# Attention, squared-ReLU layer and gated layer on one core: both layers by one level of Strassen, weights streamed from DRAM

## The reference

```python
k_p = k.reshape(B, H, Sp, 8, D).mean(axis=3); v_p = the same of v     # B, H, S, D = 8, 8, 576, 64; Sp = 72
attn = softmax(scale * q @ k_p.T) @ v_p                               # softmax over the 72 pooled keys
x = attn.transpose(0, 2, 1, 3).reshape(4608, 512)                     # 8 batches of 576 tokens
h = x @ moe_w_in                                                      # 512 x 2048
x2 = (s * relu(h) ** 2 + b) @ moe_w_out                               # 2048 x 512
h2 = x2 @ moe2_w_in                                                   # 512 x 2048
out = (h2 * sigmoid(h2)) @ moe2_w_out                                 # 2048 x 512
```

## Time and profile before

| what | value |
|---|---|
| median of 3 runs | 1729.53 us (1729.25 to 1729.66) |
| span of the profiled execution, first to last instruction | 1729.0 us |
| TensorE matmul busy | 1702.6 us, 98% |
| VectorE busy | 752.9 us, 44% |
| ScalarE busy | 568.8 us, 33% |
| GpSimd busy | 280.7 us, 16% |
| moved by DMA | 75.88 MB, 44 GB/s over the span |

### The profile page before, as it was taken

How to read it: one execution, slowest core, us unless ns; L and a number is a source line. 1 busy time by engine, 2 the same in 40 slices (tenths; PEclk the granted TensorE clock), 3 DMA queues, 4 the chain that set the end, 5 groups by cost and what they waited for, 6 DMA issues and landing times.

```text
span 1729.0 us, 22661 instructions
## 1 busy us (share of the span) xinstructions
PE 1702.6 (98%) x7894; PEld 1416.9 (82%) x7894; DVE 752.9 (44%) x1248; ACT 568.8 (33%) x1099; POOL 280.7 (16%) x374
## 2 busy tenths in 40 slices
PE   7999999999999999999999999999999999999999
PEld 6777888888888888888888888888888888888887
DVE  6666555555655555552345232323232323232322
ACT  4444333333334334332323232323232323232222
POOL 5652211222121121200077000000000000000000
PEclk9999999999999999999999999999999999999999
DMA  5431111111111111120123010101010101010000
GB/s 154 129 104 54 44 54 35 42 59 36 60 42 29 59 42 45 36 74 1 49 91 127 1 49 0 49 0 49 0 49 0 49 0 49 0 49 0 24 0 24
DMA packets 30509, 75.88 MB, mean 44 GB/s; under 512 B 7824, under 2 KB 7824, under 8 KB 27024
## 3 DMA queue, kind: packets, MB, share of 16 engines
q1 hardware_dynamic: 22848, 55.59, 10.5%
q10 hardware_dynamic: 7632, 19.93, 3.0%
HBM read 55.58 MB, written 19.92 MB: 44 GB/s over the span
## 4 chain that ended last, share of the span: by engine, by line
PE 90%; DVE 5%; issue 2%; ACT 2%; DMA 1%; POOL 0%; SPq 0%; ACTq 0%; DVEq 0%; POOLq 0%
PE y_ps L525 43%; PE h_ps L512 42%; PE a_ps L473 2%; PE a_ps L487 2%; PE a_ps L456 1%; DVE g_raw L799 1%; DVE rowmax L739 1%; ACT act L629 1%; ACT g_hi L639 1%; DVE rowsum L754 1%; DVE g_lo L811 0%; DVE probs L761 0%; DVE probs L749 0%; DMA xrest_dram<-xrest 0%; DMA x_raw<-kT 0%
## 5 line engine op out<-in xcount | busy, mean ns | idle before, releaser
L512 PE MATMUL h_ps<-x_hi,w_hi 128*128 128x512 f32 x1152 | 453.8, 394 | 4.3 <-DVE x_lo L787 3.7
L525 PE MATMUL y_ps<-g_hi,w_hi 128*128 128x512 f32 x1152 | 452.6, 393 | 0.0
L512 PE MATMUL h_ps<-x_hi,w_lo 128*128 128x512 f32 x1152 | 450.2, 391 | 0.0
L512 PE MATMUL h_ps<-x_lo,w_hi 128*128 128x512 f32 x1152 | 449.9, 391 | 0.0
L525 PE MATMUL y_ps<-g_hi,w_lo 128*128 128x512 f32 x1152 | 449.4, 390 | 0.0
L525 PE MATMUL y_ps<-g_lo,w_hi 128*128 128x512 f32 x1152 | 448.8, 390 | 0.0
L629 ACT ACTIVATE act<-h_ps 128x512 f32<-128x512 f32 x288 | 171.9, 597 | 679.2 <-PE h_ps L512 679.1
L796 DVE TENSOR_TENSOR g_raw<-h_ps,act 128x512 f32<-128x512 f32 x144 | 99.5, 691 | 411.3 <-ACT act L629 411.2
L512 PEld LDWEIGHTS h_ps<-x_hi,w_hi 128*128 128x128 f32 x1152 | 217.1, 188 | 48.2 <-issue 4.1
L512 PEld LDWEIGHTS h_ps<-x_hi,w_lo 128*128 128x128 f32 x1152 | 216.7, 188 | 45.8
L525 PEld LDWEIGHTS y_ps<-g_hi,w_lo 128*128 128x128 f32 x1152 | 216.3, 188 | 45.8
(11 more groups left out here) (106 smaller groups left out, 977.5 us busy)
## 6 DMA issues: line engine op xcount, KB each, us to landing
w_stage<-weights SPq DMA_DIRECT2D x64, 256.0 KB, 2.9
x_dram<-y_out ACTq DMA_DIRECT2D x9, 1024.0 KB, 3.9
x_raw<-x_dram SPq DMA_DIRECT2D x9, 1024.0 KB, 4.7
k_stage<-kT SPq DMA_DIRECT2D x30, 288.0 KB, 3.2
q_sb<-qT SPq DMA_DIRECT2D x30, 288.0 KB, 2.8
v_stage<-vP SPq DMA_DIRECT2D x30, 288.0 KB
out<-y_out ACTq DMA_DIRECT2D x8, 1024.0 KB, 3.9
xrest_dram<-xrest ACTq DMA_DIRECT2D x32, 32.0 KB, 1.6
```

What stands on the lines that cost most here:

```text
L512: last = nc.tensor.matmul(h_ps[f % 2][:, :], w[:, f, cols], x[:, c, :], start=(c == 0 and n == 0), stop=(c == KC - 1 and n == 2))
L525: last = nc.tensor.matmul(y_ps[m][:, :], w[:, f, cols], g[:, f % G, :], start=(f == 0 and n == 0), stop=(f == FS - 1 and n == 2))
```

## The change

One level of Strassen's scheme (in a form with operand sums T1 to T4) replaces each layer product of 2x2 quadrants, 8 block products, by 7. A unit is now one batch of 576 columns in two halves of 288 (`TH`). It goes through the first layer (an even phase `ph`) and then the second (odd), before the next batch; there are 8 units and 16 phases. A phase has 56 slots: 28 up (4 groups `g` of 7 products) and 28 down (7 products in 2 pieces of 2 slots; `d` is the slot counted from the first down slot). Each slot is 12 matmuls of 288 columns and uses one granule of weights, 128 x 1024 float32 with high and low parts. Granules are no longer kept in SBUF: a ring of 6 is loaded from `w_dram`, one per slot, in every phase. `w_dram` is filled by the kernel: 32 sets of raw weights (`load_set`, 512 KB) are summed by GpSimd (`sum_set`, 4 operations on 128x256), split by ScalarE and VectorE (`prep`, in two parts of 4x256 and 3x256 columns), and stored by SyncE (`store_set`, two DMAs that write 1 KB pieces, 1.84 MB in all). Sets 0 to 3 are made ahead of the first slot, the other 28 during slots 0 to 76 of the first unit.

In the core of each step, PSUM sums are copied by ScalarE (`part_up`, `part_down`) and combined by VectorE (`form`); the results of the function are kept in float32 for the whole phase (`gq`), where VectorE makes the operand sums (`combine`, `xsum`), ScalarE the high parts (`dhi`, `xhi`) and VectorE the low parts (`dlo`, `xlo`). The attention of batch u+1 is woven into unit u: for units 1 to 6 wholly into the 56 slots of the even phase, 14 slots for each pair.

The diff in its core; the rest is names, buffers and the matching changes of SyncE's and GpSimd's lists:

```diff
-NB = 512
+ORDER = ("P1", "P5", "P6", "P3", "P7", "P2", "P4")
+TH = 288
+DOWN = ((0, 0), (1, 0), (0, 1), (1, 1), (2, 0), (2, 1), (3, 0), (3, 1), (4, 0), (4, 1), (5, 0), (5, 1), (6, 0), (6, 1))
+PIECES = tuple(2 if i < 4 else 1 for i in range(len(DOWN)))
+RING = 6
...
+TURN_NAMES = ("scores", "sub", "exp", "sum", "norm", "turn0", "lo0", "turn1", "lo1", "values0", "add0", "values1", "add1")
+def turns_of(u):
+    if u + 1 >= B:
+        return {}
+    base, stride = (28, 14) if u == 0 else (0, 14)
+    return {base + stride * p + i: (name, (u + 1) * PAIRS + p)
+            for p in range(PAIRS) for i, name in enumerate(TURN_NAMES)}
...
+def prep_slots():
+    slots = {}
+    for m in range(2 * FIRST_SETS, 2 * NSETS):
+        at = m - 2 * FIRST_SETS if m < 32 else 24 + int((m - 32) * 1.7)
+        slots.setdefault(at, []).append(m)
+    return slots
...
# SyncE
+            def store_set(n):
...
+                sp.wait_ge(whi_ready, 2 * n + 2)
+                sp.dma_start(rows[:, :, half[0]].rearrange("j p n -> p j n"), w_hi[:, n % 2, :, :].bitcast(F32)
+                             ).then_inc(w_stored[n % 2], DMA)
+                sp.wait_ge(wlo_ready, 2 * n + 2)
+                sp.dma_start(rows[:, :, half[1]].rearrange("j p n -> p j n"), w_lo[:, n % 2, :, :].bitcast(F32)
+                             ).then_inc(w_stored[n % 2], DMA)
+            def load_gran(ph, slot):
+                n = gran(ph, slot) - 1
+                if ph < 2:
+                    for i in sets_of(slot):
+                        i += ph * 2 * SETS
+                        sp.wait_ge(w_stored[i % 2], (i // 2 + 1) * 2 * DMA)
+                if n >= RING:
+                    sp.wait_ge(gran_done, n - RING + 1)
+                sp.dma_start(ring[:, n % RING, :].bitcast(F32), w_dram[row_of(ph, slot)]).then_inc(gran_landed[n % RING], DMA)
...
# TensorE: the turns before the slot
+                elif turn in ("turn0", "turn1"):
+                    if e == 0:
+                        pe.wait_ge(normed, t + 1)
...
+                    elif t >= PAIRS:
+                        pe.wait_ge(plo_ready, 2 * t + 1)
...
+                elif turn in ("values0", "values1"):
+                    if e == 0:
+                        pe.wait_ge(v_used, t + 1)
+                        pe.wait_ge(plo_ready, 2 * t + 2)
+                    else:
+                        pe.wait_ge(x_summed, (t - PAIRS) * 2 + 1)
...
+            def up(ph, slot):
...
+                pe.wait_ge(gran_landed[n % RING], (n // RING + 1) * DMA)
...
+                for half in range(2):
+                    for k in range(2):
+                        at = half * 512 + k * P
+                        w1, w2 = ring[:, n % RING, at:at + P], ring[:, n % RING, at + 256:at + 256 + P]
+                        for i, (w, x) in enumerate(((w1, xc_hi), (w1, xc_lo), (w2, xc_hi))):
+                            last = nc.tensor.matmul(bank[:, half, 0:TH], w, x[:, j, k, :],
...
+                last.then_inc(gran_done, 1)
...
# ScalarE
+            def dhi(ph, idx, c=0):
+                (j, h), nth = DOWN[idx], ph * len(DOWN) + idx
+                old_ph, old_idx = divmod(nth - 3, len(DOWN))
...
+                if nth >= 3:
+                    act.wait_ge(gran_done, gran(old_ph, SLOTS_UP + 2 * old_idx + 1))
...
+            def down_slot(ph, d):
+                idx, c = divmod(d, 2)
+                if d == 5:
+                    part_down(ph, 0, idx)
+                elif d == 7:
+                    part_down(ph, 1, idx)
+                elif d == 11:
+                    part_down(ph, 2, idx)
...
+                elif c and idx + 3 < len(DOWN):
+                    dhi(ph, idx + 3)
...
# VectorE
+            def down_slot(ph, d):
+                idx, c = divmod(d, 2)
+                if d in (15, 19, 23):
+                    form(ph, GROUPS_UP, (15, 19, 23).index(d))
+                if d == 1:
+                    dlo(ph, 3, 0)
+                    dlo(ph, 3, 1)
+                    combine(ph, 2, 1)
+                elif c and idx + 3 < len(DOWN):
+                    dlo(ph, idx + 3)
+                if d in (3, 5):
+                    combine(ph, 4, idx - 1)
+                elif d in (7, 9):
+                    combine(ph, 6, idx - 3)
+                if ph % 2 == 0:
+                    if d == 20:
+                        xlo(ph + 1, 3)
+                    elif d == 23:
+                        xlo(ph + 1, 0)
+                        xsum(ph + 1, 1)
...
+            for ph in range(PHASES):
+                turns = turns_of(ph // 2)
+                for slot in range(SLOTS):
+                    turn, t = turns.get(ph % 2 * SLOTS + slot, (None, None))
+                    if turn in ("scores", "sub", "sum", "norm", "lo0", "lo1", "add0", "add1"):
+                        attention(turn, t)
+                    if ph < 2:
+                        for m in PREP.get(ph * SLOTS + slot, []):
+                            prep(m)
+                    if slot < SLOTS_UP:
+                        up_slot(ph, slot)
+                    else:
+                        down_slot(ph, slot - SLOTS_UP)
```

More of the change, by code:

```diff
@@ L53 @@
 DMA = 16
[L57 to L68, removed]
+ORDER = ("P1", "P5", "P6", "P3", "P7", "P2", "P4")
+OPERAND = ("B11", "T1", "T2", "B22", "T3", "B21", "T4")
+NPROD = 7
+TH = 288
@@ L88 @@
+    ("prep", 3),
+    ("lo0", 2), ("lo1", 2), ("lo0", 3), ("lo1", 3), ("prep", 4), ("prep", 5), ("prep", 6), ("prep", 7),
 ]
 FIRST_GPSIMD = [
-    ("values", 0), ("values", 1), ("keys", 2), ("keys", 3), ("values", 2), ("values", 3), ("weights", 0),
-    ("weights", 1),
-]
[L93 to L106, removed]
+    ("values", 0), ("values", 1), ("keys", 2), ("keys", 3), ("set", 0), ("set", 1), ("values", 2), ("values", 3),
@@ L166, in build @@
[L166 to L181, removed]
-        w_landed = [sem(f"w_landed{n}") for n in range(WSLOTS)]
@@ new lines, in build, with buffers, before @@
+        odd_first = dict(odd, **vp_first[1], bank_s=b_ps, bank_v=t_ps)
+        steady = dict(even, vp=vp[0:SP, :], bank_s=t_ps, bank_v=t_ps)
+        def buffers(t):
+            if t < PAIRS:
+                return odd_first if t % 2 else even_first
+            return steady
+        def before(t):
+            if t < 2:
+                return None
+            return t - 2 if t <= PAIRS else t - 1
+        raw_landed = [sem(f"raw_landed{n}") for n in range(2)]
+        w_stored = [sem(f"w_stored{n}") for n in range(2)]
@@ L532, in ffn @@
-            def ffn(layer, u, a=None):
-                for s in range(SLOTS):
-                    if a is not None and s in TURNS:
-                        attention(TURNS[s][0], Unit(a, TURNS[s][1], steady, False))
-                    f, odd = s // 2, s % 2
-                    if s >= 2 * FS:
-                        down(layer, u, s - FS - LAG)
-                    elif not odd:
-                        up(layer, u, f)
-                    elif f >= LAG:
-                        down(layer, u, f - LAG)
+                    last.then_inc(pv_done, 1)
@@ L562, in _ @@
-            with pe.Fori(BLOCKS, 2 * BLOCKS) as u:
-                ffn(1, u)
+                    for _ in range(n):
+                        nc.tensor.matmul(a_ps[1][:, 0, 0:P], ident[:, :], ident[:, :], start=True, stop=True)
+                else:
+                    attention(turn, n)
+                read = max(read, n + 1) if turn == "values" else read
+            for ph in range(PHASES):
+                turns = turns_of(ph // 2)
+                for slot in range(SLOTS):
+                    turn, t = turns.get(ph % 2 * SLOTS + slot, (None, None))
+                    if turn in ("scores", "turn0", "turn1", "values0", "values1"):
+                        attention(turn, t)
+                    if slot < SLOTS_UP:
+                        up(ph, slot)
+                    else:
+                        down(ph, slot)
@@ L829, in ffn @@
-            def ffn(layer, u, a=None, split=True):
-                for s in range(SLOTS):
-                    f, odd = s // 2, s % 2
-                    if odd and f < FS:
-                        graw_op(layer, u, f)
-                    if a is not None and s in TURNS:
-                        attention(TURNS[s][0], Unit(a, TURNS[s][1], steady, False))
-                    if odd and f < FS:
-                        lo_op(layer, u, f)
-                    if s == 2 * FS - 1 and split:
-                        split_x(u + 1)
-                y_evac(u)
```

1092 lines of the change are left out of this document (619 added, 473 removed).

## The result

The changed kernel takes 2096.8 us (median of 4 runs, 2095.91 to 2098.38), the kernel before 1729.39 (4 runs, 1728.82 to 1729.66) on the same chip: a ratio of 1.212, 95% interval 1.2105 to 1.214. The forecast was 2008 with a range of 1775 to 2130. So the direction is as forecast and the time 89 us longer.

What follows compares the result with a forecast made beforehand. The prediction took TensorE's matmuls to bound the old kernel. Start 60, slots 0 to 76 320, slots 77 to 111 57, six units of 231, last unit 179 and end 5 gave 2007, forecast 2008 us, range 1775 to 2130.

Steps and rivals of the forecast that it cites:

- TensorE's stream: All slots: 10752 matmuls of 288 columns at 133 ns each, 1430 us, 134 us less than before.
- Attention in the even phases: Units 1 to 6: TensorE waits for attention steps behind dhi, dlo and combine in VectorE's list, 33 us per phase.
- The clock: Even phases of units 1 to 6: half-speed clock after TensorE's idle stretches, 5 us per phase, 0 to 12 possible.
- The steady supply: Granule loads after unit 0: 65.7 MB per unit at 340 GB/s, under 384, so costed at nothing.
- Unit 0: Slots 0 to 76: 113 MB through the queue take 295 us, plus 25 for imperfect overlap, 320 us.
- my rate of 384: DMA in slots 0 to 76: GB/s taken from the mostly storing queue q10, giving 295 us for 113 MB.
- 187 us are waits for granules: Slots 0 to 76: TensorE needs 133 of 320 us and waits for granules the other 187.
- TensorE's largest wait is for landed granules: Expected sign in slots 0 to 76, lasting until about 380 us with DMA share near 1.0.
- rival 2: Order only: unit 0 is held by its lists, slots 0 to 76 take some 153 us, total 1841; chance 0.07.
- The start: Time to the first slot, with preparation of the first sets ahead: 60 us instead of 43, bounds 54 and 68.
- Slots 77 to 111: The other 35 slots of unit 0: 56 us and 1 for turns, 57 us.
- the 415 us of booked waits: TensorE's waits, 187 us in unit 0 and 228 in units 1 to 6; faster only if they shrink under 137.

Runs made afterwards that it cites:

- e1: The changed kernel with VectorE's attention steps norm, lo0, lo1, add0 and add1 one slot earlier in its list: 1870.91 us.
- e4: The changed kernel with 24 matmuls of 128 columns added ahead of each turn in slots 33 to 41, from the third phase on: 2092.89 us.
- e10: The changed kernel with VectorE's attention steps moved ahead and units 1 to 6's attention put in the up halves of both phases: 1849.23 us.
- e6: The changed kernel with VectorE's attention steps moved ahead and only the four starting weight sets prepared, all granules loaded from their rows: 1691.52 us.
- e7: The changed kernel with each next raw set loaded ahead of the two stores of the set just split: 2107.51 us.
- e9: The changed kernel making all 32 weight sets but storing only the first four, granules loaded from those sets' rows: 2026.64 us.

## Why the forecast came out as it did

**TensorE's stream: right.** In the down half of phase 7 ten distances take 1.32 us, 132 ns each, as the earlier trace rows say:

```profile
1146.88 0.29 PE L603 MATMUL b_ps<-sp_hi,ring 128*128 128x288 f32 x1
...
1148.20 0.30 PE L603 MATMUL b_ps<-sp_lo,ring 128*128 128x288 f32 x1
```

336 of them take 44.8 us. By the rule that the Trainium skill (TensorE: Matmul & The Clock Gate, Back-to-back issue gap) gives for the gap of an isolated matmul it would be 122.5 ns; the trace disagrees by 10 ns here too.

**Attention in the even phases: right in mechanism and place, and nearly in size.** 31.9 us per phase against 33. Its terms, in phase 2 (forecast, measured): norm 4.0, 7.5; lo0 4.2, 3.7; lo1 4.2, 3.4; add0 3.6, 2.5; in the second set of turns norm 2.3, 2.1; lo0 2.0, 1.25; lo1 2.0, 1.9; add0 5.9, 7.5. The first norm was mis-sized: the scores come at the end of the up half, where VectorE is still in that half's last burst. In the up half 3.2 us were measured for some 4. The prices at 1152 columns fit: 1372 ns plain and 1252 on ScalarE (forecast 1.37 and 1.27), 1422 with a scalar (forecast 1.54):

```profile
L923 DVE TENSOR_TENSOR gq<-gq 128x1152 f32<-128x1152 f32 x96 | 131.7, 1372 | 1.7
...
L935 DVE SCALAR_TENSOR_TENSOR sp_lo<-gq,b_col,sp_hi 128x1152 fp32r<-128x1152 f32 x48 | 68.3, 1422 | 117.2 <-ACT sp_hi L706 117.0
...
L706 ACT ACTIVATE sp_hi<-gq,b_col 128x1152 fp32r<-128x1152 f32 x48 | 60.1, 1252 | 55.1 <-PE b_ps L603 29.8 <-PE a_ps L603 25.3
```

**The clock: this term was mis-sized.** I booked 5 us per phase. The down half of phase 2 is 44.8 + 7.2 for turns + 30.7 of waits = 82.7 and takes 93.2: 10.5 us are matmuls at half clock. Over the six phases this rest is 10.5 to 14.4 us, 12.3 in the mean. Six times the 7.3 us too few are 44 of the 89 us, the largest miss of the sum. The rest goes when the waits go (1.0 us in e1); whether it can be had back while they stay is open, since in e4 the added matmuls themselves came in the way.

**The steady supply: nearly right.** Waits for granules are 4.2 us in units 1 to 7 on one line and 1.1 on another, not nothing; odd phases take 91.4 us in the mean instead of 89.4, at 328 to 344 GB/s and a DMA share of 0.92 to 0.95. That is 2 us in each of six units, of which the waits are 0.8 and the next unit's first scores, which stand ahead of its slot 0, another 1.1.

**Unit 0: the term was right in size (330 for 320), its working only in part.** I counted 113 MB; the trace has 108 in these 330 us, 328 GB/s at a DMA share of 0.97. At the 346 GB/s of the first 128 us they would take 312. So my rate of 384 was too high by a tenth or more, and the bytes counted too many and the 25 us added for the buffers made up for it, which is luck. By the Trainium skill (DMA: Bandwidth & Descriptors, Bandwidth) 358 GB/s, each core's part when both cores of a pair are at it, would give 316 us for my 113 MB, and the same section has up to 425 for a core alone. The window of 128 us at full share shows 346, closer to this than to my rate, though one of 30 us (260 to 290) shows 378. The step "187 us are waits for granules" was wrong: TensorE is busy for 186 of the 330 us, where I had 133, at a granted clock of 0.75; of its idle 144 us it waits 9.6 for granules and nearly all the rest for PSUM banks and attention turns, behind the `prep` steps in the lists of ScalarE and VectorE. The line "TensorE's largest wait is for landed granules" is refuted by the waits shown above. Two bounds lie close together: with the bytes nearly halved 280, with the stores gone 258, with the prep steps gone too 185, and with VectorE's order mended as well 147, nearly rival 2's 153. Rival 2 alone was not what happened, since at full traffic the DMA engines are full; but what it names is there, 50 us below. What share of the 73 us belongs to which of the three lists stays open: no kernel here moved the prep steps of one engine alone.

**The start was mis-sized by 10 us**, beyond its bounds of 54 and 68. The chain into slot 0 shows a part of why (start us, length, what):

```profile
56.41 1.46 SPq L324
...
57.91 1.35 SPq L307
...
59.30 1.28 SPq L313
...
61.19 8.64 DMA ring<-w_dram
...
69.97 2.26 PE a_ps L581 x8
```

Three issues took 1.3 to 1.5 us each, where the stores' issues before them took 0.36, and the first granule, behind the store and the raw set, 8.64 us.

**Slots 77 to 111** took 65.7 for 57: 4.6 us are waits for granules, which I had put at nothing there; the window has a DMA share of 0.97. The remaining 4 us are unassigned but for the last turns of attention and a clock of 0.97.

Together: 10 + 10 + 9 + 6 x 10 = 89 us over, no stretch shorter than forecast. None of them would have turned the verdict; the 415 us of booked waits had to fall under 137 for that, and the mended order takes away only some 248.

**What holds the best version.** e10 is 158 us longer than e6, and its slots 0 to 76 are 168 us longer (315.4 and 147.1). After unit 0 it runs nearly at TensorE's pace (e10, then e1's slots 0 to 76):

```profile
500.00:1800.00 1300.00, 1267.99 (x9446) 1249.66 (x9445) 955.00 (x1188) 648.49 (x887) 147.59 (x198) 1.00 0.93 328
...
70.10:385.30 315.20, 184.32 (x1029) 175.40 (x1029) 166.89 (x191) 117.66 (x154) 116.36 (x143) 0.75 1.00 339
```

The whole change moves 601.5 MB. At the 346 GB/s of the change's first 128 us these are 1738 us, at the 339 GB/s of e1's 315 us 1774, both more than the kernel before takes. This is an estimate and was not run; a higher lasting rate, of which only the 30 us at 378 GB/s is a hint, would move it.

## What to carry to other kernels

Before fewer multiplications are bought with more elementwise work, walk through each in-order list and ask what stands ahead of the step that the bound engine waits for: here the same instructions in another order are worth 226 us, while the busy shares (61% and 41%) looked harmless. A filler that is to keep an engine warm is sized by its distance in a trace: e4's was twice as long as planned, and the run could not answer its question. A stage that prepares data once still takes its bytes and its list entries, and both must fit under the work beside it: here 77 slots of 133 us took 330. Where a wait is removed next to a full queue, look for its successor: e7 turned a wait for a load into one for a store.

## What the runs showed of the hardware

Mixed loads and stores at a full DMA share moved 346 GB/s over 128 us in the change and 339 over 315 us in e1; windows of 28 to 38 us at full share lie between 328 and 378, and windows of 2 or 3 us in the kernel before show 366 and 390.

SyncE's issue of a raw set took 0.57 to 0.71 us in e6, which loads only four, and 0.57 to 5.56 in the change, 2.41 in the median of 32. Issues of granules took 0.32 in the median, of the low stores 0.37, with single ones up to 3.1 and 5.8. That the queues' fill causes this was not tested.

GpSimd's 128x256 additions took 0.72 to 0.74 us where VectorE stood still beside them (89 of 128 in the change). Where VectorE was at work for over nine tenths of the time (28 of 128) the median is 1.19 and the longest 1.84; in e9 54 of 128 took over 1.05, as here:

```profile
149.93 0.96 DVE L873 TENSOR_TENSOR w_lo<-w,w_hi 128x768 fp32r<-128x768 f32 x1 [1.28 <-ACT w_hi L668]
149.95 1.53 POOL L450 TENSOR_TENSOR w<-w 128x256 f32<-128x256 f32 x1
...
155.08 0.72 POOL L447 TENSOR_TENSOR w<-w 128x256 f32<-128x256 f32 x1 [2.39 <-DMA w<-weights]
```

Which of VectorE's operations do this was not tried. A matmul of float32 operands (not fp32r) with 128 columns stands in e4 as two records, 112 ns apart at full clock.
